# Attention, experts and a gated product on one core: one more pair with its causal masks in the bias, low parts of the last layers' weights in halves, and two moved sums

## The reference

```python
# attention: 16 heads of 576 x 64
scores = q @ k.T / 8
cum = cumsum(maximum(s, 0))
bias = -(cum[:, :, :, None] - cum[:, :, None, :])
scores = where(causal, -1e9, scores + minimum(bias, 0.0))
attn = softmax(scores) @ v
# x: 1152 tokens x 512 features. Experts: all 8 for every token
P = exp(x @ w_gate - max), then 8 rounds of row and column normalization
for e in range(8):
    out += P[:, e:e+1] * (maximum(x @ w1[e], 0) @ w2[e])     # 512 -> 1024 -> 512
# gated product, "the last layers"
a = x @ w_a;  b = x @ w_b                                    # 512 -> 1536
out = (a * b) @ w_out
```

## Time and profile before

| | us |
|---|---|
| runs, median (lowest to highest) | 1076.22 (1076.18 to 1076.35) |
| the profiled execution's own time | 1076.61 |
| its span in the profile | 1074.8 |
| TensorE busy, share of the span | 1068.5, 99% |
| granted TensorE clock | 1.0 over the span and in each stretch below |
| VectorE / ACT / POOL busy | 709.6 (66%) / 425.4 (40%) / 358.4 (33%) |
| TensorE busy in 0 to 92, attention | 89.05 of 92.00 |
| in 92 to 128, handover and first expert | 35.72 of 36.00 |
| in 128 to 838, experts | 710.00 of 710.00 |
| in 838 to 861, the turn | 23.00 of 23.00 |
| in 861 to 1075, last layers | 210.78 of 214.00 |
| list of waits: TensorE idle behind VectorE's sums (kept_c, L1347) | 0.5 |
| list of waits: TensorE idle behind the loads of k (nat<-in_k) | 0.8, 2 times |
| mask matmuls of TensorE (L1770), both pairs, mean of 16 | 0.222 |
| DMA of the bias' rows (bias<-cum_dram), issue to landing, median of 14 | 3.9 |

### The profile page before, as it was taken

How to read it: one execution, slowest core, us unless ns; L and a number is a source line. 1 busy time by engine, 2 the same in 40 slices (tenths; PEclk the granted TensorE clock), 3 DMA queues, 4 the chain that set the end, 5 groups by cost and what they waited for, 6 DMA issues and landing times. The chain is left out here.

```text
span 1074.8 us, 19205 instructions
## 1 busy us (share of the span) xinstructions
PE 1068.5 (99%) x6696; PEld 965.2 (90%) x6696; DVE 709.6 (66%) x1497; ACT 425.4 (40%) x984; POOL 358.4 (33%) x484
## 2 busy tenths in 40 slices
PE   9999999999999999999999999999999999999999
PEld 7778989989898998989899898989989899898997
DVE  7788876666475665646566564756656687586682
ACT  6988536234161423415142341514234434132220
POOL 2776604223040422304032230403224285154420
PEclk9999999999999999999999999999999999999999
DMA  8772211211111111111112121111211002102002
GB/s 190 188 175 71 60 40 40 60 40 57 42 39 39 39 59 39 59 39 39 39 39 59 39 59 39 39 40 38 59 41 59 23 23 75 40 20 79 21 1 88
DMA packets 93430, 60.06 MB, mean 56 GB/s; under 512 B 32928, under 2 KB 79776, under 8 KB 93376
## 3 DMA queue, kind: packets, MB, share of 16 engines
q1 hardware_dynamic: 92144, 59.02, 19.9%
q10 hardware_dynamic: 1232, 0.33, 0.2%
HBM read 56.94 MB, written 2.40 MB: 55 GB/s over the span
## 5 line engine op out<-in xcount | busy, mean ns | idle before, releaser
L766 POOL TENSOR_TENSOR hl<-kept_c,hh 128x320 fp32r<-128x320 f32 (+1 forms) x128 | 105.0, 821 | 524.6 <-ACT kept_c L967 524.6
L2025 PE MATMUL bank<-w2h,hh 128*128 128x512 f32 x680 | 266.2, 392 | 0.0
L2027 PE MATMUL bank<-w2h,hl 128*128 128x512 f32 x680 | 264.8, 389 | 0.0
L2026 PE MATMUL bank<-w2l,hh 128*128 128x512 f32 x680 | 264.8, 389 | 0.0
L1518 DVE SCALAR_TENSOR_TENSOR acc<-bank,P,acc 128x512 f32<-128x512 f32 x135 | 101.4, 751 | 196.1 <-PE bank L2027 196.1
L1885 PE MATMUL bank<-xh,w1h 128*128 128x320 f32 (+1 forms) x704 | 210.0, 298 | 0.6 <-DVE kept_c L1347 0.5
L1347 DVE TENSOR_TENSOR kept_c<-bank,kept_c 128x256 f32<-128x256 f32 (+1 forms) x440 | 183.8, 453 | 38.6 <-PE bank L1887 35.0
L1887 PE MATMUL bank<-xh,w1l 128*128 128x320 f32 (+1 forms) x704 | 208.3, 296 | 0.0
L1886 PE MATMUL bank<-xl,w1h 128*128 128x320 f32 (+1 forms) x704 | 208.3, 296 | 0.0
L965 ACT ACTIVATE hh<-kept_c 128x256 fp32r<-128x256 f32 (+1 forms) x256 | 113.2, 443 | 156.6 <-DVE kept_c L1347 156.6
L865 ACT ACTIVATE kept_one<-bank 128x256 f32<-128x256 f32 (+1 forms) x88 | 34.8, 396 | 322.6 <-PE bank L1887 322.5
(11 more groups left out here) (161 smaller groups left out, 1432.2 us busy)
## 6 DMA issues: line engine op xcount, KB each, us to landing
raw<-in_moe_w SPq DMA_DIRECT2D x32, 512.0 KB, 3.5
raw<-in_moe_w SPq DMA_DIRECT2D x32, 256.0 KB, 2.7
raw<-in_moe_w SPq DMA_DIRECT2D x64, 128.0 KB, 2.6
bias<-cum_dram SPq DMA_DIRECT2D x14, 256.0 KB, 3.9
raw<-in_moe_w_a SPq DMA_DIRECT2D x12, 256.0 KB, 2.8
raw<-in_moe_w_b SPq DMA_DIRECT2D x24, 128.0 KB, 2.9
raw<-in_moe_w_out SPq DMA_DIRECT2D x6, 512.0 KB, 3.8
bias_tail<-cum_dram SPq DMA_DIRECT2D x16, 144.0 KB, 4.3
```

What stands on the lines that cost most here:

```text
L766: pool.tensor_tensor(hl[:, 3 - place, columns(b, s)], src[:, 0:width(s)], hh[:, place, columns(b, s)].bitcast(F32), ALU.subtract).then_inc ...
L2025: pe.matmul(bank, hh[:, place, at], w2h[:, place, :], start=(nth == 0), stop=False)
L2026: pe.matmul(bank, hh[:, place, at], w2l[:, place, :], start=False, stop=False)
L2027: ins = pe.matmul(bank, hl[:, 3 - place, at], w2h[:, place, :], start=False, stop=(nth == 3))
```

## The change

Four edits:
1. `MASKED_FROM` is 1 in place of 2: pair 1 too has its masks in the bias, by POOL, and not by matmuls. Its block 0 is a copy that POOL makes (`tensor_copy`) and not a second DMA, which stays for pairs from 2 on (`LOADED_TWICE_FROM`). In `mask_first` the two wide operations come first (head 1, then head 0), then the others, and each result is counted, so that DVE waits for four counts per pair where it waited for one.
2. In ACT's handover order `keep_one(1, 1, 1)` stands ahead of `high_t(2, 0)` and `high_t(3, 0)`.
3. In DVE's order of the first expert the sums `c00` and `u2` of the third set stand right behind `low_w2(0)`, ahead of `low_w2(1)` and `largest()`.
4. In the last layers part 1 of the low weights (128x1024 behind `u3`) becomes two operations of 128x512: `low_sums(..., 0)` behind `c10` and `low_sums(..., 1)` behind `c01`. TensorE's wait for it is met by the second.

```diff
-    MASKED_FROM = 2
+    MASKED_FROM = 1
+    LOADED_TWICE_FROM = 2
@@ load_rows
-            if p >= MASKED_FROM:
+            if p >= LOADED_TWICE_FROM:
                 for r in range(2):
                     sp.dma_start(bias_of(z, r)[:, 0:PART],
@@ mask_first
+            for r in (1, 0):
+                blocks = bias_blocks(z, r)
+                pool.tensor_tensor(blocks[:, 1:8:6, :], blocks[:, 2:4, :], mask.broadcast_to([PART, 2, PART]),
+                                   ALU.add).then_inc(first_masked, 1)
             for r in range(2):
                 blocks = bias_blocks(z, r)
-                pool.tensor_tensor(blocks[:, 1:8:6, :], blocks[:, 2:4, :], mask.broadcast_to([PART, 2, PART]), ALU.add)
-                ins = pool.tensor_tensor(blocks[:, 6, :], blocks[:, 4, :], maskb[:, :], ALU.add)
-            ins.then_inc(first_masked, 1)
+                if p < LOADED_TWICE_FROM:
+                    pool.tensor_copy(blocks[:, 0, :], blocks[:, 2, :])
+                pool.tensor_tensor(blocks[:, 6, :], blocks[:, 4, :], maskb[:, :], ALU.add).then_inc(first_masked, 1)
@@ ACT, handover
+        keep_one(1, 1, 1, True)
         high_t(2, 0)
         high_t(3, 0)
-        keep_one(1, 1, 1, True)
@@ biased
-                if p < MASKED_FROM:
-                    dve.wait_ge(bias_loaded[z], DMA * loads_of_bias(p))
-                else:
-                    dve.wait_ge(first_masked, p - MASKED_FROM + 1)
+                dve.wait_ge(first_masked, 4 * (p - MASKED_FROM) + 1)
+            elif (t, r) in ((0, 0), (2, 0), (2, 1)):
+                dve.wait_ge(first_masked, 4 * (p - MASKED_FROM) + {(0, 0): 2, (2, 0): 3, (2, 1): 4}[t, r])
@@ DVE, next to low_w1
+        def low_sums(unit, place, half):
+
+            dve.wait_ge(w1_hi, 2 * unit + 2)
+            blocks = slice(3 + 2 * half, 5 + 2 * half)
+            ins = dve.tensor_tensor(w1l[place][:, blocks, :, :], mixed[place][:, 2 * half:2 * half + 2, :, :],
+                                    w1h[place][:, blocks, :, :].bitcast(F32), ALU.subtract)
+            if half == 1:
+                ins.then_inc(w1_lo, 1)
@@ DVE, half_of_sets
-                if not early:
+                if not (first and n < 3):
                     add_c00(i, nth, s)
-                add_u2(i, nth, s, early)
+                if not (first and n == 2):
+                    add_u2(i, nth, s, early)
...
                     low_w2(2 * e + h, c)
+                    if first and c == 0:
+
+                        add_c00(2, 2, 0)
+                        add_u2(2, 2, 0)
@@ DVE, last layers
-                for unit, part in lows:
-                    if part == 1:
-                        low_w1(UNITS + GC * g + unit, unit % 2, part)
                 if j > 0:
                     add_c11(i, n, s)
                     add_u4(i, n, s)
                     add_c10(i, n, s)
+
+                for unit, part in lows:
+                    if part == 1:
+                        low_sums(UNITS + GC * g + unit, unit % 2, 0)
                 if n in w2_at(g)[:-1]:
                     low_w2(HALVES + g, w2_at(g).index(n))
                 add_c01(i, n, s)
                 for unit, part in lows:
-
                     if part == 0:
                         low_w1(UNITS + GC * g + unit, unit % 2, part)
+                    else:
+                        low_sums(UNITS + GC * g + unit, unit % 2, 1)
```

## The result

The changed kernel takes 1077.62 us (median of 22 runs, 1076.96 to 1080.03), the kernel before 1076.18 (22 runs, 1075.44 to 1076.51): a ratio of 1.0016, interval 1.0009 to 1.0022, so 1.4 us slower, 0.16%. The forecast was 1077.2, slower by 1.0.

The account below looks back on a forecast made before the run. TensorE, busy 99% of the span, was taken as the bound. Masks -0.2, keep_one -0.28, third set +0.2 and halves +1.3 gave +1.0 us: 1077.6 profiled, 1077.2 for the median, range 1074.8 to 1078.6.

Parts of the forecast that it names:

- Halved low parts: Last layers: second half queues behind POOL's multiplication, delaying product 6 of sets 4 and 6; +1.3, bounds -1.0 and +5.
- The gains: Last layers: TensorE's stalls removed, 0.55 and 0.41 at product 2 in group 0, four of 0.17 at product 4.
- Third set: First expert: product 4 earlier by 0.35 + 0.11, lost again as second w2l queues behind POOL; +0.2, bounds -0.46 and +0.4.
- keep_one: Handover from attention: keep_one two copies earlier lets product 5 follow the transposes nearly seamlessly; -0.28, bounds -0.2 and -0.35.
- Masks: Attention, pair 1: nine short masks taken off TensorE and made by POOL; -0.2, bounds 0 and -0.5.
- the last five: Masks before later score groups of pair 1 (2, 2 and 1): a start of 0.06 each, 0.3 together, taken as -0.2.
- the first four: Masks before pair 1's second score group: no gain, since the wait for VectorE's tail step takes their place.
- Rival 3: Attention: loads of k, idling TensorE 0.8 us, decide; earlier masks may shift this, 1076.2 to 1078.2; chance 0.13.
- the sum: Whole kernel: -0.2 - 0.28 + 0.2 + 1.3 = +1.0 us, 1077.2 for the median; chance 0.62.
- Halves free of POOL: Last layers: VectorE gets in first or queueing does not hold there; -1.9, with seams -1.3, 1074.9; chance 0.17.
- first halves losing too: Last layers: POOL wins over the first halves as well, +3.7 more in six sets, 1080.9; chance 0.05.
- Masks that come late: Attention, pair 1: mask rows land behind other loads, VectorE waits up to 1 us, 1078.4; chance 0.03.

Follow-up runs that it names:

- change, twice: Changed kernel with all four edits, timed a second time beside the kernel before: 1077.62 us first, 1077.32 us again, ratio 1.0014.
- halves alone: Kernel before with edit 4 only (halves behind c10 and c01): 1077.66 us, ratio 1.0014.
- POOL held back: Kernel before with edit 4, and POOL's first multiplication in sets 3 and 5 waiting for c01 instead of c10: 1078.40 us, ratio 1.0021.
- one piece behind c10: Kernel before with part 1 of the low weights still whole (128x1024), moved from behind u3 to behind c10: 1075.67 us, ratio 0.9996.
- +0.4 alone: Kernel before with edit 1 only (pair 1's masks in its bias): 1076.45 us, ratio 1.0003.
- the combination: Kernel before with edits 2, 3, maximum before second w2l, whole low part behind c10, fourth set's c00 between low parts, weights' load later: 1074.78; plus edit 1: 1074.62.
- keep_one and the sums: Kernel before with edits 2 and 3 only: 1076.14 us, ratio 1.0000.
- order of halves: Kernel before with halves behind c10 and c01 (edit 4): 1077.66 us; or with halves behind u3 and u4, ahead of c10: 1076.45 us.

## Why the prediction was right

**Halved low parts, the largest term.** Forecast +1.3, measured +1.2 (change, twice), +1.38 (halves alone). By parts: set 4 of group 0, 0.85 + 0.11 forecast, 0.85 + 0.10 measured; sets 4 and 6 of groups 1 and 2, 0.28 + 0.11 forecast, 0.31 + 0.10 measured; set 6 of group 0, 0.40 forecast, 0.31 measured (0.43 with the halves alone). The gains came as forecast too: the stalls of the earlier trace rows are gone. What carried it was the arithmetic of the earlier trace rows, where an operation with both inputs in SBUF and a POOL operation do not share but queue; the second half was to take 0.97, and took 0.97. The run with POOL held back shows that it is POOL that makes the halves long: 680 ns for 825. It does not show the whole price that way, since its own wait brings new stalls; that comes from the one piece at the first half's place, which has no stall at product 6 in groups 1 and 2. The page SBUF — State Buffer of the Trainium skill (section Who interferes with whom) calls the port pair that the two share an exclusive lock, and says that the order of issue decides who blocks; the trace agrees, first halves at 0.68 with POOL asking 0.16 behind, second ones at 0.97 with VectorE behind.

**Third set.** Forecast +0.2; measured +0.23 by the starts of the same matmuls in both traces: product 4 comes 0.35 + 0.10 earlier, the small matmul and those behind it lose 0.51, and product 4 of the fourth set another 0.17. The second w2l was to take 1.26 and took 1.25. The wait moved from product 4 to the matmul behind it, as forecast.

**keep_one.** Forecast -0.28. By the same starts TensorE is 0.34 further on at product 5, and 0.21 to 0.22 from the transposes behind it on (100.46) up to the third set. With the third set the stretch is 34.73 us, where it was 34.72: -0.22 and +0.23.

**Masks.** Forecast -0.2, all of it from the last five; the first four were to gain nothing. The medians show little of this (+0.4 alone, -0.16 on the combination, both inside the noise). The profiles fall in two kinds, those in which pair 0's second score group comes at about 10.0 us and those from 10.5 on. Steps between second score groups, in us:

| kind, masks of pair 1 | profiles | pair 0 to pair 1 | pair 1 to pair 2 |
|---|---|---|---|
| 10.0, by TensorE (before) | 5 | 5.99 to 6.31 | 11.11 to 11.12 |
| 10.0, in the bias | 1 | 6.08 | 10.88 |
| 10.5 and later, by TensorE | 4 | 5.98 to 6.00 | 11.11 |
| 10.5 and later, in the bias (change, twice) | 4 | 5.73 | 11.13 to 11.17 |

In the first kind it is as forecast: 0.22 behind pair 1's second group, from the last five. In the second, the changed kernel's own, it is the other way round: 0.26 ahead of that group, from the first four, and nothing from the other five. The kernel with keep_one and the sums and the changed kernel show why the first four gain there:

```profile
15.73 0.52 DVE L1277 CUSTOM_DVE_ANT_0 scores_tail<-bank,bias_tail,neg_max 128x288 f32<-128x288 f32 x1
...
16.25 0.40 PE L1775 MATMUL bank<-maskb,identb 128*128 128x128 bf16 x4
16.57 0.45 PE L1763 MATMUL bank<-qk 64*128 64x384 f32 x2
```

```profile
15.66 0.52 DVE L1282 CUSTOM_DVE_ANT_0 scores_tail<-bank,bias_tail,neg_max 128x288 f32<-128x288 f32 x1
```

The masks begin when VectorE's tail step has ended (16.25) and not 0.36 ahead of its end as in the earlier trace rows, so the wait for the bank hides nothing of them; without them the scores of the changed kernel start at 16.25, 0.07 behind its tail's end (16.18). The size of this term is right, but that it is right in the changed kernel is in part luck, since the step of the working that gave the first four nothing, and the five all, holds only in the other kind. Why the five give nothing there stays open.

**Loads.** Rival 3 gave attention 0.13 for a shift either way. In the first profile they cost 0.29 more than in the kernel before's, in the second nothing (10.91). What they do to a median no run separates.

**What the sum left out.** The forecast's +1.0 stands against 1.3 and 1.4 in the medians. Inside the span it is met as far as medians can say, which leave about 1 us open either way: 1075.2 against 1074.2 in the second measurement. The other 0.35 lies outside the span, in every run of the changed kernel, and the sum had no term for it: it took what lies between span and time as unchanged. Its cause stays open. The highest runs of the changed kernel, up to 1080.03 where before never passed 1076.75, no run here explains either; the 1080.03 has a granted clock of 0.998, the only run on record below 1.0, and halves alone had one of 1079.31 at 1.0.

**The rivals.** Halves free of POOL would have shown second halves of 0.68, first halves losing too 0.9 or more: the rows exclude both. Masks that come late are excluded by POOL's first at 13.53, wanted at 16.86. The page Perfetto Trace Analysis of the Trainium skill (section Optimizing Scalar/DVE Operations) has it that breaking up instructions may let work complete sooner where VectorE is not saturated. Neither order of halves did: +1.2 and +0.56 us in the last layers, where the same work in one piece, moved behind c10, gave -0.67; VectorE is busy 66% of the span.

## What to carry to other kernels

Before splitting an operation so that urgent work can go between its parts, ask who else waits for that urgent work: here the sum ahead of the halves (c10) also released POOL's multiplication, and the second half queued behind it. Moving the whole operation to the place where the first half went cost nothing of this and gained. And where two sums, a copy and a low part must all be done by one deadline, compute each consumer's wanted time anew after removing the stall ahead of it; two of the misses among the experiments' sizes (one piece behind c10, POOL held back) came from keeping the old one. Last, compare the runs' spans and not only their times: here a quarter of the loss lay outside the span, where no reading of the trace could find it.

## What was not expected of the hardware

The loads of one pair in attention (128 KB and less each) stalled TensorE by 0 to 1.14 us in otherwise equal executions, with issues of 0.63 to 3.02 us for the same small DMA; this, and whether pair 0's scores start at 10.0 or 10.5 us, is most of what a single profile of attention differs by. The stretch behind the handover repeated to 0.1 us in every kernel whose edits lay elsewhere (944.37 to 944.46 in five), so a stall of 0.1 us there can be read from one profile where the run times cannot resolve 1 us.
